# The closing of the kernel's block: with GpSimd's drain, and joined by semaphores alone

## The chip, the cores and the metric

The kernel runs on one core of a Trainium2 chip. Its time is the device time of one execution in microseconds (us), and a kernel's figure is the median over several executions. A profile is taken of one execution more; its span goes from the first to the last instruction that the profiler recorded on the core, and the execution that was profiled also has a device time of its own.

## The reference

Three parts follow one another. `B, S, D` are 4, 576 and 512; there are 8 heads of 64, and 8 experts of width 1024.

```
# 1. linear attention: softmax of q over the head dimension, of k over the sequence
kv  = einsum('bhsd,bhse->bhde', softmax(k, axis=2), v)
x   = einsum('bhsd,bhde->bhse', softmax(q, axis=-1), kv)      # -> [B, S, D]
# 2. mixer: across the tokens, then across the channels (hidden width 1536)
u   = x + (relu(x^T @ w_tok1) @ w_tok2)^T
x1  = u + relu(u @ w_ch1) @ w_ch2
# 3. one expert of eight for each token
logits = x1 @ w_gate;  local = sigmoid(x1 @ w_local)
e[s]   = argmax(logits[s]) if s == 0 or local[s] < 0.5 else e[s-1]
out[s] = softmax(logits[s])[e[s]] * (relu(x1[s] @ w1[e[s]]) @ w2[e[s]])
```

## The kernel before

The first two parts of the reference go batch by batch. Attention and the token mixing give `u`, kept as a high and a low half, and the channel mixing is a long row of matmuls of 128 by 288 (L572) over three products of such halves. SP stores the rows of `x1` to HBM.

In the third part the tokens are sorted by expert into tiles of 128 rows. For each tile GpSimd gathers the rows with an indirect DMA (L1613), TensorE transposes them and runs the two layers of the expert (L693 and L718, with transposes at L705), ScalarE and VectorE split what it left into halves, VectorE scales the result (`yo`, L1481), and GpSimd scatters it to the output with an indirect DMA (L1625). Both kinds of indirect DMA go through the one software queue, and nothing else in the kernel does.

The number of tiles is known only at run time. The loops over the tiles on PE, ACT, DVE and POOL therefore run to the largest number there can be, load a flag from a table at every turn, and skip the tile if the flag is zero. GpSimd's loop is the longest of them in time, and after it stands the kernel's own wait for all that GpSimd moved:

```
            with pool.Fori(EARLY, NT) as t:
                live = pool.value_load(table[0:1, 3, bass.ds(t + 1, 1)], min_val=0, max_val=1)
                with pool.If(live):
                    tile(t, True)

            n = pool.value_load(tiles[0:1, 0:1], min_val=1, max_val=NT)
            pool.wait_ge(x_in, 16 * n + 32)
            pool.wait_ge(rows_stored, 16 * n)
```

`x_in` counts the gathers that have landed and `rows_stored` the scatters, 16 for each. These two waits are GpSimd's last work in its body; L1660 to L1662 are their lines. They stay as they are.

Of the kernel before, what the change touches and what calls it, by code (L numbers as in the profile page):

```python
# [36 lines left out]
def build(nc, q, k, v, w_tok1, w_tok2, w_ch1, w_ch2, w_gate, w_local, w1, w2, out):  # L37
# [42 lines left out]
    with ExitStack() as ctx:  # L80
# [239 lines left out]

            return bank[7] if early(n) and g else bank[3]

        block = ctx.enter_context(nc.Block())

        @block.sync
# [1363 lines left out]
```

## Time and profile before

| what | value |
|---|---|
| device time, median of 3 executions | 794.91 us (794.33 to 796.45) |
| device time of the profiled execution | 790.27 us |
| its span | 788.6 us |
| TensorE matmul, busy | 749.5 us, 95% of the span |
| VectorE, ScalarE, GpSimd, busy | 40%, 30% and 18% of the span |
| DMA | 61.80 MB, 78 GB/s over the span |

Busy time is that of compute instructions. Register, branch, semaphore, drain and DMA-issuing instructions are not counted in it, and they appear only where a line is asked for by itself, or as an engine's queue (POOLq, DVEq) in the chain that ended last. A stretch in which no engine is busy can thus still be full of instructions.

### The profile page before, as it was taken

Reading aid. Unit: us, or ns where it says so; the run is one execution under the profiler, and the core shown is the slowest. Engines: PE = TensorE matmul, PEld = TensorE weight load, DVE = VectorE, ACT = ScalarE, POOL = GpSimd, SP = SyncE. Lnnn points to the kernel's source line nnn. Section 1 sums busy time; section 2 is a strip of 40 time slices with the busy share of each in tenths; the row PEclk is TensorE's granted clock in tenths of the full one; section 3 lists DMA queues with packets and bytes.
Section 4 is the critical chain, followed back from the end, with each engine's and each line's share of the span. In section 5 each row is a group of like instructions: output and inputs, shape, how many; then the busy total and the mean of one; then the engine's idle time right before and its main releaser. Section 6 shows DMA issues by size and latency. Waiting matters only on the chain.

```text
span 788.6 us, 14829 instructions
## 1 busy us (share of the span) xinstructions
PE 749.5 (95%) x4836; PEld 678.5 (86%) x4837; DVE 316.6 (40%) x611; ACT 234.1 (30%) x409; POOL 142.4 (18%) x162
## 2 busy tenths in 40 slices
PE   6999999999999999999999999996999999997993
PEld 6879999999999999999999999874888888875882
DVE  6746241225332235332225424762522622257450
ACT  3743042023132023133021141313422522255340
POOL 6562020002020002020000023111221221211220
PEclk9999999999999999999999999999999999999998
DMA  9932122012131012100010510105360620136400
GB/s 210 378 66 59 33 68 54 1 32 61 31 81 41 1 32 62 31 21 11 1 35 1 196 62 16 62 28 190 118 230 34 211 90 26 36 134 210 155 27 2
DMA packets 69514, 61.80 MB, mean 78 GB/s; under 512 B 51484, under 2 KB 53244, under 8 KB 69472
## 3 DMA queue, kind: packets, MB, share of 16 engines
q1 hardware_dynamic: 65952, 51.77, 22.2%
q0 software_dynamic: 3520, 9.44, 3.5%
q8 instruction: 30, 0.49, 0.3%
q14 instruction: 12, 0.10, 0.0%
HBM read 52.99 MB, written 10.31 MB: 80 GB/s over the span
## 4 chain that ended last, share of the span: by engine, by line
PE 80%; DVE 6%; issue 3%; DMA 3%; POOL 2%; ACT 2%; SPq 2%; DVEq 1%; ACTq 0%; POOLq 0%
PE bank L572 36%; PE bank L718 13%; PE bank L693 12%; PE bank L514 5%; PE bank L543 4%; POOL qb L1577 2%; PE bank L705 2%; PE bank L537 2%; PE bank L486 2%; DMA x_rows<-x1n 1%; PE bank L593 1%; PE bank L502 1%; PE bank L582 1%; PE bank L524 1%; PE bank L641 1%
## 5 line engine op out<-in xcount | busy, mean ns | idle before, releaser
L572 PE MATMUL bank<-u_h,wc_h 128*128 128x288 f32 x384 | 120.0, 312 | 1.5 <-DVE hid_l L1303 1.5
L718 PE MATMUL bank<-wslots,hT_h 128*128 (+1 forms) x336 | 107.5, 401 | 10.1 <-DVE hT_l L1470 10.1
L572 PE MATMUL bank<-hid_h,wc_h 128*128 128x288 f32 x384 | 117.0, 305 | 0.0
L693 PE MATMUL bank<-wslots,xgT_h 128*128 (+1 forms) x344 | 111.8, 406 | 4.2 <-DVE wslots L1454 3.1
L572 PE MATMUL bank<-hid_l,wc_h 128*128 128x288 f32 x384 | 113.2, 295 | 0.0
L572 PE MATMUL bank<-u_l,wc_h 128*128 128x288 f32 x384 | 113.1, 295 | 0.0
L572 PE MATMUL bank<-u_h,wc_l 128*128 128x288 f32 x384 | 113.0, 294 | 0.0
L572 PE MATMUL bank<-hid_h,wc_l 128*128 128x288 f32 x384 | 113.0, 294 | 0.0
L1303 DVE SCALAR_TENSOR_TENSOR hid_l<-bank,hid_h 128x288 fp32r<-128x288 f32 x96 | 43.3, 454 | 132.4 <-ACT hid_h L872 132.2
L718 PEld LDWEIGHTS bank<-wslots,hT_h 128*128 128x128 f32 x336 | 62.1, 191 | 23.5 <-issue 10.8
L693 PEld LDWEIGHTS bank<-wslots,xgT_h 128*128 128x128 f32 x344 | 61.0, 188 | 17.9 <-issue 7.0
L872 ACT ACTIVATE hid_h<-bank 128x288 fp32r<-128x288 f32 x96 | 38.9, 408 | 123.4 <-PE bank L572 123.4
L572 PEld LDWEIGHTS bank<-u_h,wc_h 128*128 128x128 f32 x384 | 72.1, 188 | 2.9 <-DVE hid_l L1303 1.8
L572 PEld LDWEIGHTS bank<-u_l,wc_h 128*128 128x128 f32 x384 | 72.2, 188 | 0.7
L572 PEld LDWEIGHTS bank<-hid_l,wc_h 128*128 128x128 f32 x384 | 72.2, 188 | 0.5
L572 PEld LDWEIGHTS bank<-hid_h,wc_h 128*128 128x128 f32 x384 | 72.0, 188 | 0.6
L572 PEld LDWEIGHTS bank<-hid_h,wc_l 128*128 128x128 f32 x384 | 72.3, 188 | 0.0
L572 PEld LDWEIGHTS bank<-u_h,wc_l 128*128 128x128 f32 x384 | 72.0, 188 | 0.0
L693 PE MATMUL bank<-wslots,xgT_l 128*128 (+1 forms) x172 | 67.4, 392 | 0.0
L718 PE MATMUL bank<-wslots,hT_l 128*128 (+1 forms) x168 | 66.3, 394 | 0.0
L1310 DVE TENSOR_TENSOR x1T<-bank,u_h 128x288 f32<-128x288 f32 x32 | 14.6, 457 | 117.2 <-PE bank L572 117.2
L1577 POOL TENSOR_TENSOR qb<-qb,qmax 96x768 f32<-96x768 f32 x12 | 17.6, 1471 | 231.2 <-DVE qmax L1072 231.2
(236 smaller groups left out, 1090.2 us busy)
## 6 DMA issues: line engine op xcount, KB each, us to landing
w1raw<-in_moe_w_dram SPq DMA_DIRECT2D x24, 512.0 KB, 4.6
w2raw<-in_moe_w_dram SPq DMA_DIRECT2D x24, 512.0 KB, 6.4
wc_raw<-in_moe_w_ch_dram SPq DMA_DIRECT2D x8, 768.0 KB, 11.2
x_rows<-x1n SPq DMA_DIRECT2D x24, 192.0 KB, 2.1
kb<-in_k_dram SPq DMA_DIRECT2D x24, 144.0 KB, 3.1
qb<-in_q_dram SPq DMA_DIRECT2D x24, 144.0 KB, 3.1
vb_e<-in_v_dram SPq DMA_DIRECT2D x16, 144.0 KB, 3.6
vb_o<-in_v_dram SPq DMA_DIRECT2D x16, 144.0 KB, 3.4
```

Source lines behind the costliest of these rows:

```text
L486: last = pe.matmul(k_bank(n, g)[:, c * KV:(c + 1) * KV], keys(n)[:, i, c * P:(c + 1) * P], vb[g][:, 2 * c:2 * c + 2, i, :], start=(i == 0) ...
L514: last = pe.matmul(mix_bank(n, g)[:, c * TOK:(c + 1) * TOK], queries(n)[:, i, c * P:(c + 1) * P], wt1[:, i, :], start=(i == 0), stop=(i == ...
L537: pe.matmul(bank[4 + j % 2][:, 0:HS], kvd[:, c // CG, c % CG, :], qT[:, c // CG, c % CG, part], start=True, stop=False)
L543: last = pe.matmul(bank[4 + j % 2][:, 0:HS], h1T[:, m, c * P:(c + 1) * P], wt2[:, m, part], start=False, stop=(m == KT - 1))
L572: last = pe.matmul(to, lhsT, rhs, start=(m == 0), stop=(m == len(mms) - 1))
L693: last = pe.matmul(bank[half][:, :], xgT[a][:, c, :], w1s[x][:, bass.ds(n & 1, 1), c, half * 512:(half + 1) * 512].rearrange("p a n -> p ( ...
L705: last = pe.transpose(bank[2 + half][:, c * P:(c + 1) * P], hs[:, f * P:(f + 1) * P], ident[:, :])
L718: last = pe.matmul(bank[5][:, :], hT[a][:, f, :], w2s[x][:, bass.ds(n & 1, 1), f, :].rearrange("p a n -> p (a n)"), start=(f == 0 and (a, ...
L872: act.activation(hid[0][:, i, :], bank[idx % 2][:, 0:HS], ACT.Relu).then_inc(hid_hi, 1)
L1303: dve.scalar_tensor_tensor(out=hid[1][:, i, :], in0=psum, scalar=0.0, in1=hid[0][:, i, :], op0=ALU.max, op1=ALU.subtract).then_inc(chan_do ...
L1310: dve.tensor_tensor(x1T[:, i, :], psum, u[0][:, i, part], ALU.add).then_inc(y_sum, 1)
L1577: pool.tensor_tensor(by_head(queries(n))[:, IHALF[part], :, :], x[:, IHALF[part], :, :], by[:, IHALF[part], :].unsqueeze(3).broadcast_to([ ...
```

## The change

```
-        block = ctx.enter_context(nc.Block())
+        block = ctx.enter_context(nc.Block(no_gpsimd_drain=True))
```

## Rows read from the trace of the kernel before

**Rows 1.** The page's head: span, busy share of each engine, 40 slices.

```profile
span 788.6 us, 14829 instructions
...
PE 749.5 (95%) x4836; PEld 678.5 (86%) x4837; DVE 316.6 (40%) x611; ACT 234.1 (30%) x409; POOL 142.4 (18%) x162
...
PE   6999999999999999999999999996999999997993
```

**Rows 2.** The chain that ended last, from 740 us on: start, length, what.

```profile
773.11 2.73 PE bank L718 x12
...
776.07 0.76 DVE yo L1481
...
777.76 0.98 POOL out_dram L1625
```

**Rows 3.** Busy time by stretch: PE, PEld, DVE, ACT, POOL, PEclk, DMA share, GB/s.

```profile
650.00:775.00 125.00, 118.45 (x563) 95.10 (x562) 53.54 (x61) 49.62 (x71) 24.89 (x36) 1.00 0.27 94
775.00:779.00 4.00, 0.83 (x4) 0.37 (x2) 0.75 (x1) 0.00 (x0) 1.03 (x1) 1.00 0.00 0
779.00:788.60 9.60, 0.00 (x0) 0.00 (x0) 0.00 (x0) 0.00 (x0) 0.00 (x0) 0.59 0.02 5
```

**Rows 4.** GpSimd's loop, flag load and last wait, by line: ns min/median/max, starts.

```profile
L1655 POOLq COMPARE_BRANCH  x24: 40/45/45, 558.4 to 783.7; - x24
...
L1656 POOLq TENSOR_LOAD <-table x24: 282/292/497, 535.2 to 783.0; - x24
...
L1660 POOLq TENSOR_LOAD <-tiles x1: 298/298/298, 783.8 to 783.8; - x1
...
L1662 POOLq EVENT_SEMAPHORE  x1: 17/17/17, 784.5 to 784.5; - x1
```

**Rows 5.** The block's end, L80: duration ns min/median/max, first and last start.

```profile
L80 POOLq EVENT_SEMAPHORE  x2: 17/17/17, 788.4 to 788.5; - x2
L80 SPq DRAIN  x1: 117/117/117, 735.9 to 735.9; - x1
L80 ACTq DRAIN  x1: 8/8/8, 779.3 to 779.3; - x1
L80 PEldq DRAIN  x1: 8/8/8, 781.6 to 781.6; - x1
L80 DVEq DRAIN  x1: 17/17/17, 783.3 to 783.3; - x1
L80 POOLq COMPARE_BRANCH  x1: 38/38/38, 784.5 to 784.5; - x1
L80 POOLq DRAIN  x1: 3667/3667/3667, 784.7 to 784.7; - x1
...
L80 PEldq EVENT_SEMAPHORE  x1: 51/51/51, 788.5 to 788.5; - x1
```

**Rows 6.** GpSimd's scatters and gathers, by line: issue, and time to landing.

```profile
L1625 POOL DMA_INDIRECT out_dram<-yo,id_out x21: 1022/1028/1035, 509.1 to 777.7; - x21
...
DMA to landing us min/median/max: 2.3/2.8/7.5
...
L1613 POOL DMA_INDIRECT xg<-x_rows,id_in x23: 1023/1048/1654, 448.8 to 768.3; - x23
```

**Rows 7.** DMA activity from 784.7 to 788.3 us.

```profile
DMA packets 0, 0.00 MB, mean 0 GB/s; under 512 B 0, under 2 KB 0, under 8 KB 0
```

**Rows 8.** The barrier at the program's start, L1678, where GpSimd's drain stands too.

```profile
L1678 POOLq DRAIN  x1: 192/192/192, 0.4 to 0.4; - x1
...
L1678 SPq EVENT_SEMAPHORE  x1: 17/17/17, 0.8 to 0.8; - x1
```

**Rows 9.** Instruction fetches over the span: packets, MB, share of 16 engines.

```profile
q8 instruction: 30, 0.49, 0.3%
```

## The prediction

> **What bounds the kernel now.** I read the page's head first. TensorE is busy 95% of a span of 788.6 us, and every slice but a few shows it at 90% or more [rows 1]; a change that touches no matmul can only win in the few places where TensorE is not what the end waits for. So the second view is the chain that ended last, read from its end. Its last matmuls begin at 773.11 us, VectorE's scaling of the last tile follows at 776.07, and the chain closes with the scatter of that tile, from 777.76 for 0.98 us [rows 2]. That is 778.74, but the span ends at 788.6. The reader is to see that gap: almost 10 us at the end are on no row of that chain. The third view, the busy time by stretch, shows why: from 779 to 788.6 no engine has any compute instruction [rows 3]. What stands there is of the kinds that the page does not count, so the fourth view is that of single lines, GpSimd's loop and the block's end.
>
> They fill the gap in two pieces. Up to 783.7 GpSimd's loop runs through its remaining turns, each with a flag load of about 0.29 us and a skip; the load of the tile count is at 783.8, and the last of the kernel's own waits at 784.5, 17 ns long, since what it waits for is long there [rows 4]. Then comes the block's end: GpSimd's branch at 784.5, its drain at 784.7 with 3667 ns, its two semaphore instructions at 788.4 and 788.5, and the release of the others at 788.5, the last of them 51 ns long on TensorE [rows 5]. At the end, then, the execution waits for one thing: GpSimd's drain.
>
> **Is the drain a wait for something else?** If it waited for a transfer, taking it away would leave the transfer. The last scatter was issued at 777.7, and scatters land 2.3 to 7.5 us after issue [rows 6], so by 785.2 at the latest; the kernel's own wait for exactly that count already passed at 784.5 [rows 4], and from 784.7 to 788.3 not one DMA packet moved [rows 7]. The other engines aren't awaited either: their drains stand at 735.9, 779.3, 781.6 and 783.3, all ahead of GpSimd's [rows 5]. The 3.67 us are the instruction's own, and nothing lies beside them.
>
> **The change part by part.**
>
> *Removed: GpSimd's drain.* The next instruction, the wait for the four others, begins at 788.4, and without the drain it could begin where the drain did, at 784.7. That is 788.4 - 784.7 = 3.7 us: 3.667 of the drain and some 0.05 behind it [rows 5]. All of it is on the path that sets the end. Bounds: at most 3.8 (rounding of the two starts). At least, if only the part went that the same drain has where no software DMA was issued before it, 0.192 us as at the start of the program [rows 8], and the rest were work that something else must then do. I take 3.7, because the row is this very instruction in this place; the 0.2 stays as the other end.
>
> *Added: one semaphore instruction each on SP, ACT, DVE and PE*, where the increment rode on the drain before. The nearest rows are 17 to 51 ns [rows 5]. VectorE is the last of the four, at 783.3 + 0.02; with 0.05 more it is there by 783.4, and GpSimd comes to the barrier at 784.6 or 784.7. The cover is 1.2 us, against at most 0.05. Cost nothing; with the cover gone, 0.05.
>
> *GpSimd's side of the barrier.* It keeps a wait for four counts and a release; they stay at 784.7 and 784.8, and the four others follow within 0.1, as at 788.5. If the new barrier takes one instruction more on GpSimd, 0.02 to 0.1 us (17 ns, and about 0.08 from one of its semaphore instructions to the next, estimated from 788.4 to 788.5 [rows 5]). I take 0, and 0.1 as the bad end.
>
> *Not touched:* the waits on landed gathers and scatters, the turns of the loops, and the barrier at the start. What is late next is GpSimd's own loop: it goes on to 783.7 while the last data was out at 778.74.
>
> **Sum.** Span: 788.6 - 3.7 = 784.9 us. The profiled execution's own time is 790.27, 1.7 more than its span; with that unchanged, 786.6. The median of the executions shown is 794.91, 4.6 above the profiled one. Nothing in the trace says where those 4.6 lie, and I carry them over unchanged: 794.9 - 3.7 = **791.2 us**, or 0.47% less. A difference of 0.3%, 2.4 us, is about what a measurement of this kernel can tell from no change, so the gain is only half as large again as that bound.
>
> The Trainium skill has a figure that speaks against a gain of this size: "VectorE: DVE Perf Modes", section "The DRAIN you can't avoid", tells of boilerplate drains of about 12 ns, constant, on all five engines. Of the drains at the block's end three rows agree roughly with 8, 8 and 17 ns, and GpSimd's with 3667 ns does not [rows 5]. By the page's figure the edit would be worth 0.01 us and the time would stay at 794.9; by the row it is 791.2, and I go by the row.
>
> **The rivals.**
>
> *B: the work comes back where the span doesn't show it.* What GpSimd does in those 3.67 us goes over its software queue, and the same instruction costs 0.192 us at the start, before the first of 23 gathers and 21 scatters [rows 6, 8]. If it puts that queue in order, someone may have to do so anyway: whatever closes the execution behind the span, or the drain at the start of the next one, which would then grow from 0.192 towards 3.7. For it: the large difference between the two drains, and the 1.7 us outside the span and the 4.6 us without a row. Against it: no row shows an instruction that depends on the drain, and no transfer is open. From 1.3 us returned on, of the 3.7, the gain is below 0.3%; with all of it returned the time is 794.9. The page "Runtime: NRT & Kernel Launch" of the Trainium skill, section "The launch sequence", lists behind the kernel a barrier over the engines and a reset of the DMA rings, the latter with about 2 us; no row here shows either. By that rule the reset is done anyway and could be where the queue's work is waited for, and the time would be this rival's.
>
> *C: an instruction fetch falls into the closing.* The closing's instructions change in number and so where pages of code end. A fetch of code takes 0.003 x 16 x 788.6 / 30 = 1.3 us (estimated from the instruction queue's share of 16 engines and its 30 packets [rows 9]). On VectorE it would end at 783.3 + 1.3 = 784.6, when GpSimd arrives, and cost nothing; on GpSimd it would be in the open: 791.2 + 1.3 = 792.5, just at the bound. For it only that addresses move; against it that GpSimd gets fewer instructions, not more.
>
> *D: slower.* The undrained queue is cleared by a costlier way, DMA by DMA. The drain's price is (3.667 - 0.192) / 44 = 0.08 us for each of the 44 indirect DMAs [rows 5, 6, 8]. Slower by more than 0.3% needs more than 3.7 + 2.4 = 6.1 us for clearing, 0.14 us a DMA; at 0.16, twice the drain's, it is 7.0 us, or 791.2 + 7.0 = 798.2. It would lie outside the span or in the opening barrier. Nothing in the trace speaks for a price other than the drain's own, and the 1.7 us outside the span leave little room in the profiled execution now.
>
> That the option changes nothing isn't likely: the drain with its 3667 ns stands under the block's end [rows 5], which is what the option names. I count it to B, since it gives the same time.
>
> **How the numbers follow.** The forecast has 0.68, B 0.22, C 0.05, D 0.05. Of the forecast's 0.68 I put 0.04 within 0.3%, because the three executions shown spread over 2.1 us and the gain stands only 1.3 us over the bound; C is split evenly. So faster 0.66, within 0.3% 0.04 + 0.22 + 0.03 = 0.29, slower 0.05. The time is the forecast's, 791.2. The range begins at 790.0: the lowest execution shown less the most that the drain can give is 794.33 - 3.8 = 790.5, and half a microsecond for a median that moves by itself. It reaches to 794.9, with C and the whole of B up to the unchanged time in it; D and what of B lies above stay out.
>
> **What the profile of the changed kernel would show.** No drain of GpSimd at the block's end; its wait for the others about 0.1 us after the branch, near 784.7; the release within 0.3 us of that; a span of 784.9; drains of the four others as before, each with a semaphore instruction behind it, the last of VectorE at 783.4. The loop turns, the last scatter and all of the stages before stay where they are. B would show in the profile as a span shorter by 3.7 with the execution's own time less than 3.7 shorter, or a longer drain of GpSimd in the first microsecond. C would show as an instruction packet after 781 and a gap ahead of one engine's last instructions. The prediction is wrong if the difference of the medians is below 2.4 us while the span is shorter by 3.7, or if the span itself doesn't shrink.

## The result, and the profile after

| | kernel before | changed kernel |
|---|---|---|
| median of 20 executions | 794.93 us (789.86 to 799.25) | 790.61 us (786.24 to 794.41) |
| ratio of the times, 95% interval | 1 | 0.9946 [0.9927, 0.9964] |
| profiled execution, and its span | 790.27, 788.6 us | 791.55, 789.8 us |
| end of the last scatter's issue to end of span | 9.9 us | 6.1 us |

The changed kernel is 0.54% faster, 4.3 us, with the interval from 0.36% to 0.73%. The forecast was 3.7 us and 791.2. Yet its profiled execution is longer than that of the kernel before, 791.55 for 790.27 us. Whoever compares the two pages alone would read a change for the worse, so the first question is where each span goes.

The block's end in the changed kernel, line L80, answers to [rows 5] (durations in ns, minimum, median, maximum, then first and last start in us):

```profile
L80 SPq EVENT_SEMAPHORE  x2: 17/17/17, 740.9 to 789.8; - x2
L80 ACTq EVENT_SEMAPHORE  x2: 17/17/17, 784.6 to 789.8; - x2
L80 PEldq EVENT_SEMAPHORE  x2: 51/51/51, 786.6 to 789.8; - x2
L80 DVEq EVENT_SEMAPHORE  x2: 21/21/21, 788.3 to 789.8; - x2
L80 POOLq EVENT_SEMAPHORE  x2: 17/17/17, 789.6 to 789.7; - x2
...
L80 DVEq DRAIN  x1: 17/17/17, 788.2 to 788.2; - x1
L80 POOLq COMPARE_BRANCH  x1: 38/38/38, 789.5 to 789.5; - x1
```

No drain of GpSimd is left. The other four engines have two semaphore instructions each where they had one: the first takes the place of the increment that rode on their drain, the second is the release. VectorE's is in at 788.3, 1.2 us ahead of GpSimd's branch, the cover that the prediction gave it.

The chain that ended last shows the last scatter, which answers to the last row of [rows 2]:

```profile
782.69 0.98 POOL out_dram L1625
```

It ends at 783.67, and the span 6.1 us later. Before, it ended at 778.74 and the span 9.9 us later, so the tail is 3.7 us shorter, the term of the sum. What is left of it is, for the most part, GpSimd's six empty turns, one every 1.03 us (their flag loads, duration and first and last start; the first of them lies beside the scatter's issue):

```profile
L1656 POOLq TENSOR_LOAD <-table x6: 289/292/299, 782.7 to 787.9; - x6
```

The rest of the span, up to the last scatter, is 4.9 us *longer*, in a kernel whose engines run the same instructions up to there. Busy time by stretch shows where most of that came in. First the changed kernel (columns as in [rows 3]), then the kernel before in the same stretches and where its trace is at the second one:

```profile
17.90:24.70 6.80, 6.70 (x36) 6.69 (x37) 3.32 (x3) 2.33 (x5) 2.65 (x2) 0.50 0.98 327
...
724.50:727.90 3.40, 3.37 (x9) 2.33 (x8) 0.35 (x1) 1.23 (x2) 0.00 (x0) 0.50 0.01 5
```

```profile
17.90:24.70 6.80, 6.19 (x50) 5.79 (x51) 5.40 (x6) 3.07 (x6) 2.71 (x2) 1.00 1.05 318
...
719.60:723.00 3.40, 3.17 (x13) 2.35 (x14) 1.05 (x1) 1.22 (x2) 0.00 (x0) 1.00 0.00 0
```

The sixth figure behind the stretch's length (the numbers in brackets are counts) is the granted clock of TensorE. In both stretches it stood at 0.50, that is 1.2 GHz, in the changed kernel's execution and at 1.00, 2.4 GHz, in the other; 36 matmuls were done in the first where the other did 50.

Where the changed kernel's execution falls behind can be followed along the two traces. Up to the first stretch the two run alike, and behind it the changed kernel's is 3.2 us late (ScalarE's L804 at 24.02 and 27.21 us), where half the clock for 6.8 us gives 3.4. At the first scatter (509.12 and 512.74) it is 3.6 late, and from the fourth (558.54 and 562.70) on 4.2. The second stretch makes it 5.5 late (the transposes of L705 at 724.35 and 729.87), and 0.6 of that is given back at once, because TensorE then waits 1.0 us for VectorE where it waits 1.6 in the other trace. That leaves the 4.9. The 1.0 us that came in between the two stretches has no cause in these rows; a third stretch at 1.2 GHz, of 7 us near 550, is in both traces. Of the nine profiled executions of the whole kernel in this study, eight have a stretch at 1.2 GHz near 20 us and one near 725. The only one with neither is that of the kernel before.

The executions differ from one to the next, with either kernel, and the longer ones mostly have the lower mean clock. Of the 20 of the changed kernel the fastest, 786.24 and 786.25 us, have a mean granted clock of 0.991 and 0.993, and the slowest, 794.41, has 0.981. The profile of before was one of the faster ones of its kernel. What can be compared between two profiles here is the tail, where TensorE does nothing, and the medians of many executions, not the two spans.

### The profile page after: what moved, and what is told of

Same layout as the page of the kernel before. It is cut to its first block, busy times and chain, and to the rows that moved or that the text cites. A ratio compares the mean times of both kernels' runs of the same rounds, so it can differ in the third digit from the quotient of the medians.

```text
span 789.8 us, 14832 instructions
## 1 busy us (share of the span) xinstructions
PE 755.9 (96%) x4836; PEld 684.2 (87%) x4837; DVE 316.7 (40%) x611; ACT 234.1 (30%) x409; POOL 142.5 (18%) x162
## 3 DMA queue, kind: packets, MB, share of 16 engines
q0 software_dynamic: 3520, 9.44, 3.5%
## 4 chain that ended last, share of the span: by engine, by line
PE 81%; DVE 6%; DMA 3%; issue 2%; POOL 2%; ACT 2%; SPq 2%; DVEq 1%; ACTq 0%; POOLq 0%
PE bank L572 36%; PE bank L718 13%; PE bank L693 12%; PE bank L514 5%; PE bank L543 4%; POOL qb L1577 2%; PE bank L486 2%; PE bank L705 2%; PE bank L537 2%; DMA x_rows<-x1n 1%; PE bank L502 1%; PE bank L593 1%; PE bank L582 1%; PE bank L524 1%; PE bank L641 1%
## 6 DMA issues: line engine op xcount, KB each, us to landing
kb<-in_k_dram SPq DMA_DIRECT2D x24, 144.0 KB, 3.1
qb<-in_q_dram SPq DMA_DIRECT2D x24, 144.0 KB, 3.1
vb_e<-in_v_dram SPq DMA_DIRECT2D x16, 144.0 KB, 3.7
vb_o<-in_v_dram SPq DMA_DIRECT2D x16, 144.0 KB, 3.6
```

## The experiments

Beside each measured ratio stands the time of the kernel before, measured on the same chip. The times are medians of 4 to 12 executions, and of 12 or 17 for the kernel before; where one execution was measured, the text says so. "The tail" is always the time from the end of the last scatter's issue to the end of the span.

**A drain of its own, in the changed kernel.** The gain could be the drain's, or come from the form of the barrier or from code that moved.

```
             pool.wait_ge(rows_stored, 16 * n)
+            pool.sem_inc(xg_cleared, 1)
+            pool.drain()
```

> The changed kernel, with a drain on GpSimd written at the end of its own body, one semaphore increment behind the last wait; the block still closes by semaphores alone. Theory A (the drain instruction itself costs 3.7 us on the path): a GpSimd drain of 3.6 to 3.7 us again, 9.8 to 9.9 us from the end of the last scatter to the end of the span where the changed kernel has 6.1 and the kernel before 9.8, and a time within 0.2% of the kernel before. Theory F (the gain came from the form of the barrier, or from code that moved): the drain is short, or the time stays near the changed kernel's, 0.5% below the kernel before.

Measured: 794.99 us against 794.68, ratio 1.0003 [0.9987, 1.0018]. The line of the added drain:

```profile
L1664 POOLq DRAIN  x1: 3671/3671/3671, 789.6 to 789.6; - x1
```

The tail is 793.5 - 783.8 = 9.7 us, where the changed kernel has 6.1. With the drain back, and the barrier still made of semaphores alone, the whole gain is gone. Theory A holds and F falls: the barrier's form is worth nothing that can be measured.

**Two drains in a row, in the kernel before.** The same two lines, added to the kernel before. What does the instruction do in 3.67 us when no transfer is open?

> The kernel before, with one more drain on GpSimd directly ahead of the block's own. Nothing is issued between the two. Theory G (fixed price of each drain once the software queue was used): both take 3.6 to 3.7 us, 13.6 us from the last scatter to the end of the span. Theory H (price of what was issued since the last drain, 0.08 us for each of 44 DMAs): the first takes 3.67, the second about 0.2, and the end of the span is 10.1 us behind the last scatter.

Measured (one execution, 792.9 us): the added drain, and the block's own right behind it.

```profile
L1664 POOLq DRAIN  x1: 3671/3671/3671, 787.2 to 787.2; - x1
```

```profile
L80 POOLq DRAIN  x1: 34/34/34, 790.9 to 790.9; - x1
```

The second one costs 34 ns, and the tail is 791.2 - 781.4 = 9.8 us, where the kernel before has 9.9. Theory G, a fixed price for each drain, is out. The first drain does work that the second one finds done.

**A drain ahead of GpSimd's loop.** One drain after 8 indirect DMAs (5 gathers, 3 scatters), added to the kernel before; 36 more follow it up to the block's own.

```
+            pool.sem_inc(xg_cleared, 1)
+            pool.drain()
             with pool.Fori(EARLY, NT) as t:
```

> The kernel before, with one more drain on GpSimd ahead of its loop over the tiles, after 5 gathers and 3 scatters; its own drain at the block's end stays, with 36 DMAs behind the first. Theory G (fixed): both 3.6 to 3.7 us, the first somewhat longer where a DMA has still to land. Theory H (by DMA): the first 0.2 + 8 x 0.08 = 0.8 us and whatever it waits for a landing, the second 3.0 us. Both: the first lies in GpSimd's idle time and costs the execution nothing that one look can show.

Measured (one execution, 794.65 us): first the added drain, then the block's own.

```profile
L1656 POOLq DRAIN  x1: 3319/3319/3319, 539.0 to 539.0; - x1
```

```profile
L80 POOLq DRAIN  x1: 3005/3005/3005, 789.7 to 789.7; - x1
```

The closing one fell from 3667 to 3005 ns, to just the 3.0 us that the price by DMA gives, and the tail is 9.2 us. The first drain was to take 0.8 us by the count and took 3.3. It began while GpSimd had not yet issued the third scatter:

```profile
539.10 1.03 POOL L1625 DMA_INDIRECT out_dram<-yo,id_out  x1 [3.59 <-DVE yo L1481]
```

That scatter landed some 2.8 us after 539.10, at 541.9, and the drain ended at 542.3. So it also waits for what is still to be issued and to land; how much of the price by DMA is paid beside that wait is not told apart.

**The drain by itself.** A kernel of its own, with GpSimd alone and the computation left out: it scatters rows of ones and drains behind each group. The code is shortened to the order of its steps.

```
for i in range(18): pool.memset(tiles[i][:, :], 1.0).then_inc(set_up, 1)
pool.iota(at[:, :], ...); wait for all; pool.drain()   # L55: no DMA yet
scatter(1);  pool.drain()                              # L81
             pool.drain()                              # L83
scatter(4);  pool.drain()                              # L85
scatter(16); pool.drain()                              # L87
scatter(44); pool.drain()                              # L89
plain(1);    pool.drain()                              # L91
plain(16);   pool.drain()                              # L93
scatter(1, wait=False); pool.drain()                   # L95
```

> A kernel of its own that leaves all of the computation out: GpSimd alone, rows of ones scattered to the output by indirect DMAs of 128 rows, then plain DMAs, with a drain behind each group, and each group landed before its drain except the last. Drains in order: after compute instructions and no DMA; after 1 scatter; directly again; after 4 more; after 16; after 44; after 1 plain DMA; after 16 plain; after 1 scatter that has not been waited for; and the block's own at the end. Theory G (fixed once the queue was used): 0.2, then 3.6 to 3.7 each whatever the count, the unwaited one up to 2 us more. Theory H (by DMA since the last drain, 0.08 us each): 0.2, 0.3, 0.2, 0.5, 1.5, 3.7, 0.3, 1.5, then 0.3 and the wait, 0.2.

Measured, line by line (L41 is the block's own drain, behind a memset and no DMA):

```profile
L55 POOLq DRAIN  x1: 46/46/46, 9.4 to 9.4; - x1
...
L81 POOLq DRAIN  x1: 126/126/126, 13.4 to 13.4; - x1
L83 POOLq DRAIN  x1: 34/34/34, 13.6 to 13.6; - x1
L85 POOLq DRAIN  x1: 378/378/378, 21.1 to 21.1; - x1
L87 POOLq DRAIN  x1: 1354/1354/1354, 46.5 to 46.5; - x1
L89 POOLq DRAIN  x1: 3631/3631/3631, 115.3 to 115.3; - x1
L91 POOLq DRAIN  x1: 119/119/119, 121.9 to 121.9; - x1
L93 POOLq DRAIN  x1: 1351/1351/1351, 138.4 to 138.4; - x1
L95 POOLq DRAIN  x1: 2995/2995/2995, 140.4 to 140.4; - x1
L41 POOLq DRAIN  x1: 299/299/299, 143.8 to 143.8; - x1
```

From 1 to 44 scatters the drain grows by (3631 - 126) / 43 = 81.5 ns a DMA, from 1 to 16 by 81.9, and for plain DMAs by (1351 - 119) / 15 = 82.1. With none it is 34 to 46 ns where GpSimd has nothing else to finish. That each group had landed beforehand doesn't change it: the price is for DMAs issued since the last drain, of either kind. It doesn't go by their bytes: 44 DMAs cost 3631 ns here with 11.54 MB and 3667 ns in the kernel before with 9.44 MB. Each of these DMAs has 128 rows and 80 packets, so a price by row or by packet fits as well as one by DMA, and no run tells them apart.

For the scatter that was not waited for, the drain lasts until it lands:

```profile
140.57 1.02 POOL L63 DMA_INDIRECT out_dram<-tile,at  x1 [5.06 <-issue]
```

It landed 2.8 us after 140.57, at 143.4, and there the drain that began at 140.4 ends. Of its 2995 ns some 1.0 is GpSimd's own issue of that scatter. Theory H holds in its slope, 0.082 us a DMA where 0.08 was expected. Its base was too high: seven of the eight rows up to L93 came out 0.12 to 0.18 us below what was expected and the eighth, after 44, 0.07 below, because I took 0.2 us for an empty drain where it is 0.04. The 192 ns at the program's start [rows 8] may be a wait for GpSimd's own work: the last memset ahead of that drain ends at 0.54 us and the drain at 0.6. So may the 299 ns at the end of this kernel, behind a memset that ends at 144.0.

**A drain in every turn of the loop, in the kernel before.** If the price goes by DMA, a kernel that needs the closing drain can pay it beforehand where GpSimd idles.

```
                 with pool.If(live):
+                    pool.drain()
                     tile(t, True)
```

> The kernel before, its closing drain kept, with a drain on GpSimd at the start of every one of the 18 live turns, where GpSimd has idle time. By the price by DMA (0.082 us each since the last drain) the closing drain has 2 DMAs left: 0.2 us, and the end of the span is 6.3 us behind the last scatter. The drains in the turns wait for the scatter before them to land, 1 to 3 us each, in time in which GpSimd would wait for VectorE anyway: time 3.5 us below the kernel before, as the changed kernel. Rival: a gather is issued up to 3 us later for it and TensorE waits for its rows; then the time is above the changed kernel's, up to 18 x 1 us.

Measured: 790.98 us against 794.39, ratio 0.9961 [0.9947, 0.9976]. The drains in the turns, and the closing one:

```profile
L1658 POOLq DRAIN  x18: 2068/2174/7592, 538.4 to 768.8; - x18
```

```profile
L80 POOLq DRAIN  x1: 216/216/216, 787.4 to 787.4; - x1
```

The closing drain has 2 DMAs left and takes 216 ns. The tail is 787.8 - 781.5 = 6.3 us, as expected. The 18 in the turns took 49 us of GpSimd's time together, most of them 2.1 to 2.2 us and the longest 7.6, which is more than the 3 us that were expected at most. Yet the execution got *shorter* by 3.4 us, and the intervals of this run and of the changed kernel overlap. TensorE waited for gathered rows once, for 0.8 us, where it was 0.9 in the kernel before. Only the drain at the end was on the path.

**The empty turns of the loop.** In the changed kernel most of the tail of 6.1 us is GpSimd's six empty turns and the load of the tile count. The four loops over the tiles now end at the number of tiles that was counted. First with the drain kept, in the kernel before, then in the changed kernel; the same edit for `pe`, `act`, `dve` and `pool`:

```
-            with pool.Fori(EARLY, NT) as t:
+            n_tiles = pool.value_load(tiles[0:1, 0:1], min_val=EARLY + 1, max_val=NT)
+            with pool.Fori(EARLY, n_tiles) as t:
```

> The kernel before, its drain kept, with the four loops over the tiles ending at the number of tiles that was counted (loaded once ahead of each loop) where they ran to the largest possible one: 18 turns for 24. Theory: the six empty turns lie on the path behind the last scatter, and now the landing of the last scatter bounds: it lands 1.3 us behind the end of its issue, then 0.4, then the drain with 44 x 0.082 = 3.7 us in the open. From the last scatter to the end of the span 5.5 us for 9.8, time 4.3 us or 0.5% below the kernel before. Rival: the drain overlaps the landing or waits with it, and the tail is 4 us; or the turns hid the drain's work in part, and it gets longer by as much as they get shorter.

> The changed kernel with the same bound on the four loops. Both are needed for the shortest end: from the last scatter to the end of the span 1.7 to 1.9 us (6.1 in the changed kernel), which is 3.7 less than with the drain kept. Time 3.7 + 4.3 = 8.0 us below the kernel before, ratio 0.990. Rival: the load of the bound ahead of TensorE's loop, 0.5 us, is on TensorE's path and takes some of it back, ratio 0.9905; or the kernel's end is held by something that the empty turns covered, VectorE or TensorE, and the tail stays over 3 us.

Measured: with the drain kept 790.74 us against 794.39, ratio 0.9954 [0.9941, 0.9968]; without it 786.28 us, ratio 0.9897 [0.9880, 0.9913]. The end of the chain and the block's end, with the drain kept:

```profile
783.95 0.82 POOL out_dram L1628
```

```profile
L80 PEldq DRAIN  x1: 2720/2720/2720, 779.2 to 779.2; - x1
...
L80 DVEq DRAIN  x1: 603/603/603, 782.3 to 782.3; - x1
L80 POOLq COMPARE_BRANCH  x1: 43/43/43, 786.1 to 786.1; - x1
L80 POOLq DRAIN  x1: 3664/3664/3664, 786.3 to 786.3; - x1
```

and without it:

```profile
781.99 0.82 POOL out_dram L1628
```

```profile
L80 POOLq COMPARE_BRANCH  x1: 43/43/43, 784.2 to 784.2; - x1
```

The tails are 790.2 - 784.8 = 5.4 us and 784.6 - 782.8 = 1.8 us, close to the 5.5 and the 1.7 to 1.9 that were expected. In the tails the two edits add up: 9.9 - 5.4 = 4.5 us from the turns and 5.4 - 1.8 = 3.6 from the drain. In the medians it is 3.7 and 4.5, together 8.1 us where 8.0 were expected; with 4 to 6 executions each, the difference of 0.8 between the two splits is within the scatter. The drain did not overlap the landing, since the kernel's own wait stands ahead of it.

**Without the flag in each turn.** With the bound, the flag's load and branch in every turn can go, in the changed kernel with the bound.

```
             with pool.Fori(EARLY, n_tiles) as t:
-                live = pool.value_load(table[0:1, 3, bass.ds(t + 1, 1)], min_val=0, max_val=1)
-                with pool.If(live):
-                    tile(t, True)
+                tile(t, True)
```

> The changed kernel with the bound on the four loops and without the flag's load and branch in each turn, which the bound makes needless. Each turn's sequencer work is 0.6 us shorter on four engines. Theory: all of it lies beside waits for TensorE's matmuls, so the time is that of the kernel with the bound alone, ratio 0.990, within 0.1%. Rival: TensorE's own queue is late at the turn of a tile, and 18 turns give up to 18 x 0.1 = 2 us more.

Measured: 786.83 us against 794.39, ratio 0.9904 [0.9888, 0.9921], no different from the bound alone. What the flags of the live turns may cost is below what these four executions can show. The shortest kernels of the study are thus the changed one with the bound on the four loops, with the flags or without, some 1.0% below the kernel before.

## Why the prediction was right, point by point

**What the end waits for: right.** The path behind the last scatter held GpSimd's turns and its drain. Taking the drain out shortened the tail by 3.7 us, putting it back made it 3.6 longer again, and moving its work under idle time saved as much as dropping it, within the intervals.

**"The 3.67 us are the instruction's own": right, and now with a content.** It is 44 DMAs at 0.082 us and some 0.04 for the instruction itself. No open transfer and no other engine was behind it.

**Added semaphore instructions and GpSimd's side at nothing: right.** VectorE was at the barrier 1.2 us early, and GpSimd's first barrier instruction stands 0.1 us behind its branch, where the drain stood 0.2 behind it.

**The sum: right in its term, with some luck in the total.** 3.7 us were forecast and 4.3 measured, with an interval of 2.9 to 5.8 us that holds the forecast. The tail has just the 3.7; the other 0.6 us of the medians has no cause that a run shows, and is within their scatter. The same scatter decides how close 790.61 comes to 791.2: it stands 0.6 us above the low end of the range, which was set from the lowest of only three executions, 794.33, while the lowest of 20 was 789.86.

**The span of 784.9 us: wrong.** It was 789.8, longer than the 788.6 before, and the last scatter did not stay at 777.7 but came at 782.7. By the prediction's own sign, "if the span itself doesn't shrink", it would have been wrong. It was the sign that was ill chosen. It compares one execution with one other, which differ by more than the 3.7 us up to the last scatter; the part of the span that the change touches, the tail, shrank as forecast. And the one profiled execution that it starts from was among the fastest of its kernel.

**The 4.6 us between the profiled execution and the median: rightly carried over, and now placed.** The prediction said that nothing in the trace tells where they lie. In the changed kernel's 20 executions the time is 1.7 us above the span every time (1.66 to 1.77), and in the 29 executions of the kernel before that were measured with the experiments likewise (1.65 to 1.78). So the 4.6 us are in the span itself. The mean granted clock goes with them: it is 0.991 in the profiled execution, and 0.978 to 0.987 in those 29, which are all longer.

**Rival B, the work comes back elsewhere: out, as far as these runs go.** Time and span stay 1.7 us apart in the changed kernel as in the kernel before, so nothing was added behind the span. The drain at the program's start is as it was, answering to [rows 8]:

```profile
L1678 POOLq DRAIN  x1: 193/193/193, 0.4 to 0.4; - x1
```

That row alone would not be enough, since it isn't known which kernel ran ahead of that execution. But had the work come back in the time of the changed kernel's own executions, the gain of the medians would be below the 3.7 us of the tail. It is 4.3, and by its interval at least 2.9, so that at most 0.8 us of the drain's work could have come back unseen. The 1.7 and 4.6 us that were counted for this rival were no evidence for it. The reset behind the kernel, about 2 us with the barrier before it, that the page "Runtime: NRT & Kernel Launch" of the Trainium skill lists in "The launch sequence" is shown by no run here; if there is one, it took no more time behind the changed kernel than behind the other.

**The 12 ns for a drain.** The section "The DRAIN you can't avoid" of the page "VectorE: DVE Perf Modes" of the Trainium skill speaks of the boilerplate ahead of and behind a kernel; the prediction asked what it would make of the drains at a block's end. On TensorE, ScalarE and VectorE with nothing left to finish they are of that size, 8 to 17 ns. It does not hold for SyncE, 117 ns, for GpSimd, where the price goes by DMA, nor for TensorE with matmuls before it: 2720 ns in the kernel whose loops end at the bound. The measurement decides.

**Rival C, a code fetch in the closing: not on the path.** One instruction packet moved at 785.5 us, but one did at 780.2 in the kernel before as well, and no engine has a gap for it at the block's end. **Rival D** had nearly the right price, 0.08 us a DMA (measured 0.082; its 0.19 us for an empty drain was too high), and the wrong consequence: no time shows that anyone else pays it.

## What to carry to other kernels

Look behind the last row of the chain that ended last: where the span goes on for microseconds and no engine is busy, ask for the lines of the block's end and of the loops, since drains, flag loads and branches are counted as busy nowhere. Here a GpSimd drain cost 0.08 us for each DMA of 128 rows that GpSimd issued since the last one, even if all had landed. This kernel waits on its own semaphores for all of them, so that no DMA was open where the drain stood, and the drain could be left out. Where it is kept, its work can be spread over GpSimd's idle time. And don't compare two spans that differ by less than the executions of one kernel do: compare the stretch that the change touches.

## What the runs showed of the hardware that was not expected

- A GpSimd drain is linear in the DMAs issued since the last, 81.5 to 82.1 ns each between 1 and 44 (all of 128 rows), indirect or plain, on top of some 40 ns; a second drain right behind it took 34 ns.
- A drain on TensorE took 8 ns when empty turns of a loop lay between it and the last matmul, and 2720 ns when it stood right behind the loop, from 779.2 to 781.9, where the last matmul ends too; on VectorE 17 and 603 ns, up to 782.9, where its last instruction ends. The empty turns had hidden this too, and it stayed off the path, as GpSimd came last.
- The granted clock of TensorE fell to 1.2 GHz for a stretch near 20 us and one near 725 us in eight profiled executions, while in another of the same instructions it stayed at 2.4 GHz in both. The times of one kernel spread over some 8 us, twice what the change was worth, and the longer executions mostly have the lower mean clock. That mean can't be compared between the kernels either: in the kernel before, from 784.0 us to the end, with TensorE idle, it stands at 0.50, and the change shortens that tail.
